# Attention: the denominators of a head in one addition on GpSimd and one inversion on VectorE

## The reference

```python
mask = q_bucket[:, :, :, None] == k_bucket[:, :, None, :]
scores = scale * np.matmul(q, k.transpose(0, 1, 3, 2))
scores = np.where(mask, scores, -1000000000.0)
scores = scores - np.max(scores, axis=-1, keepdims=True)
attn = np.exp(scores)
attn = attn / (np.sum(attn, axis=-1, keepdims=True) + 1e-09)
return np.matmul(attn, v).astype(np.float32)
```

## Time and profile before

| | us |
|---|---|
| median of 3 runs | 746.81 (746.05 to 746.90) |
| the profiled execution | 748.6 |
| its span | 746.8 |
| TensorE, busy in the span | 720.7 (97%) |
| VectorE | 570.9 (76%) |
| ScalarE | 499.9 (67%) |
| GpSimd | 320.1 (43%) |

### The profile page before, as it was taken

How to read it: one execution, slowest core, us unless ns; L and a number is a source line. 1 busy time by engine, 2 the same in 40 slices (tenths; PEclk the granted TensorE clock), 3 DMA queues, 4 the chain that set the end, 5 groups by cost and what they waited for, 6 DMA issues and landing times. The chain is left out here.

```text
span 746.8 us, 13137 instructions
## 1 busy us (share of the span) xinstructions
PE 720.7 (97%) x4017; PEld 608.5 (81%) x4017; DVE 570.9 (76%) x944; ACT 499.9 (67%) x916; POOL 320.1 (43%) x289
## 2 busy tenths in 40 slices
PE   5999999999999989999999999999999999999996
PEld 4889888989998768888888878778887888878884
DVE  6989999999999665629993181498888787887874
ACT  6878788888887653549993272566666656666562
POOL 7767566778741460000000000055454754557543
PEclk9999999999999999999999999999999999999999
DMA  3811111104133368418992000132322423225221
GB/s 128 289 48 39 57 37 47 59 18 160 40 119 128 104 183 285 166 66 313 353 366 84 0 29 0 29 109 88 92 104 85 153 100 100 99 86 169 84 81 60
DMA packets 40532, 85.05 MB, mean 114 GB/s; under 512 B 5585, under 2 KB 9841, under 8 KB 40497
## 3 DMA queue, kind: packets, MB, share of 16 engines
q1 hardware_dynamic: 37776, 77.01, 30.3%
q0 software_dynamic: 2000, 6.98, 2.9%
q10 hardware_dynamic: 720, 0.64, 0.2%
HBM read 76.82 MB, written 6.68 MB: 112 GB/s over the span
## 5 line engine op out<-in xcount | busy, mean ns | idle before, releaser
L601 POOL TENSOR_TENSOR hres<-hexp,hres 128x512 f32<-128x512 f32 x46 | 59.6, 1297 | 305.7 <-DVE hres L1268 305.7
L668 ACT ACTIVATE pTh<-psA 128x384 fp32r<-128x384 f32 x192 | 83.9, 491 | 39.3 <-PE psA L1376 39.0
L949 DVE TENSOR_TENSOR pTl<-psA,pTh 128x384 fp32r<-128x384 f32 x192 | 97.7, 551 | 9.3 <-ACT pTh L668 8.3
L1370 PE MATMUL psA<-K,Q 128*128 128x384 f32 x384 | 92.9, 365 | 3.7 <-ACT K L705 1.7
L942 DVE TENSOR_SCALAR_CACHE_REDUCE psA<-psA 128x768 f32<-128x768 f32 x96 | 91.9, 957 | 3.7 <-PE psA L1370 3.7
L659 ACT ACTIVATE probs<-psA,negmax 128x768 f32<-128x768 f32 x96 | 87.3, 910 | 2.9 <-DVE psA L942 2.5
L1222 DVE TENSOR_TENSOR wil<-rawi,wih 128x512 fp32r<-128x512 f32 x48 | 79.2, 1651 | 6.6 <-ACT wih L787 6.6
L859 ACT ACTIVATE habs<-psA 128x512 f32<-128x512 f32 x48 | 28.7, 598 | 76.8 <-PE psA L1632 74.8
L1206 DVE SCALAR_TENSOR_TENSOR hTl<-psA,hTh 128x512 fp32r<-128x512 f32 x32 | 21.5, 689 | 73.6 <-ACT hTh L767 73.3
L1376 PEld LDWEIGHTS psA<-ident_r,probs_bits 128*128 128x128 f32 x576 | 59.6, 144 | 17.1 <-issue 7.5
L604 POOL TENSOR_TENSOR hsum<-hsum,hres 128x512 f32<-128x512 f32 x46 | 69.7, 1514 | 8.2 <-POOL hres L601 8.2
(11 more groups left out here) (243 smaller groups left out, 1661.1 us busy)
## 6 DMA issues: line engine op xcount, KB each, us to landing
w2s<-in_moe_w SPq DMA_DIRECT2D x9, 2048.0 KB, 10.1
w1s<-in_moe_w SPq DMA_DIRECT2D x9, 2048.0 KB, 10.3
rawi<-in_moe_w_in SPq DMA_DIRECT2D x48, 256.0 KB, 2.6
rawo<-in_moe_w_out SPq DMA_DIRECT2D x48, 256.0 KB, 2.7
raw<-in_qk SPq DMA_DIRECT2D x16, 384.0 KB, 3.2
vs<-in_v SPq DMA_DIRECT2D x16, 192.0 KB, 2.4
x_rows<-X SPq DMA_DIRECT2D x1, 1728.0 KB, 6.8
x_rows<-X SPq DMA_DIRECT2D x1, 1512.0 KB, 5.5
```

Source lines behind the costliest of these rows:

```text
L668: nc.scalar.activation(pTh[u // TPGR % 2][:, g * TPH:(g + 1) * TPH, u % TPGR * P:(u % TPGR + 1) * P], psA[2][:, g, 0:HALF].rearrange("p (t ...
L949: V.tensor_tensor(pTl[u // TPGR % 2][:, g * TPH:(g + 1) * TPH, cols], psA[2][:, g, 0:HALF].rearrange("p (t n) -> p t n", t=TPH), pTh[u // ...
L1370: last = T.matmul(psA[u % 2][:, h, 0:HALF], qs[par][:, cols], ks[par][:, h * HALF:(h + 1) * HALF], start=start, stop=not start)
```

## The change

`den` and `inv` get six columns. GpSimd adds 1e-9 to a head's six sums in one instruction, `denominators`, after `split_qk` of the head two further on (within `prepare`, so between L506 and L474); for heads 13 and 14 it stands at the end of GpSimd's attention work. It waits for the exponentials, for its own split, and for the inversion of the head before. VectorE waits for it and inverts six numbers in the first of a head's two normalisations; the second one only multiplies. For head 15 VectorE does the addition itself. The semaphore `den_step` gives way to `den_ready` and `inv_ready`.

```diff
-        den = sb("den", [P, TPGR])
-        inv = sb("inv", [P, TPGR])
+        den = sb("den", [P, TPB])
+        inv = sb("inv", [P, TPB])
@@ gpsimd
+            def denominators(i, par, before):
+
+                wait_reg(exp_done, i * TPB + TPB)
+                wait_reg(k_split, before)
+                if not (type(i) is int and i == 0):
+                    wait_reg(inv_ready, i)
+                pool.tensor_scalar(den[:, :], sums[:, par * TPB:(par + 1) * TPB], 1e-9, None, ALU.add).then_inc(den_ready, 1)
+                wait_reg(den_ready, i + 1)
+
             def prepare(i, par):
                 split_qk(i, par)
+                if not (type(i) is int and i < 2):
+                    denominators(i - 2, par, i + 1)
                 scale(i + 1, 1 - par)
                 split_v(i, par)
...
             split_qk(HEADS - 1, 1)
+            denominators(HEADS - 3, 1, HEADS)
             split_v(HEADS - 1, 1)
+            wait_reg(v_split, HEADS)
+            denominators(HEADS - 2, 0, HEADS)
@@ vector, normalise
-                dve.wait_ge(exp_done, G * TPGR + TPGR)
-                V.tensor_scalar(den[:, :], sums[:, gm * TPGR:(gm + 1) * TPGR], 1e-9, None, ALU.add).then_inc(den_step, 1)
-                dve.wait_ge(den_step, G * 2 + 1)
-                V.reciprocal(inv[:, :], den[:, :]).then_inc(den_step, 1)
-                dve.wait_ge(den_step, G * 2 + 2)
+                if type(G) is int and G == PAIRS - 2:
+                    dve.wait_ge(exp_done, HEADS * TPB)
+                    V.tensor_scalar(den[:, :], sums[:, TPB:2 * TPB], 1e-9, None, ALU.add).then_inc(den_ready, 1)
+                head = G // 2 if type(G) is int else (G - gm) // 2 + gm // 2
+                if gm % 2 == 0:
+                    dve.wait_ge(den_ready, head + 1)
+                    V.reciprocal(inv[:, :], den[:, :]).then_inc(inv_ready, 1)
+                    dve.wait_ge(inv_ready, head + 1)
                 dve.wait_ge(out_done, G + 1)
                 V.tensor_tensor(X[:, n:n + TPGR, bass.ds(col, XROW)],
                                 ps7[:, 0:TPGR * XROW].rearrange("p (t d) -> p t d", d=XROW),
-                                inv[:, :].unsqueeze(2).broadcast_to([P, TPGR, XROW]), ALU.mult).then_inc(x_ready, 1)
+                                inv[:, gm % 2 * TPGR:(gm % 2 + 1) * TPGR].unsqueeze(2).broadcast_to([P, TPGR, XROW]), ALU.mult
+                                ).then_inc(x_ready, 1)
```

More of the change, by code:

```diff
@@ L249, in build @@
         out_done = sem("out_done")
-        den_step = sem("den_step")
+        den_ready, inv_ready = map(sem, ("den_ready", "inv_ready"))
         x_ready = sem("x_ready")
```

## The result

The changed kernel took 749.1 us (748.1 to 749.5, eleven runs) against 746.8 (745.6 to 747.4, eleven runs) of the kernel before: ratio 1.0026, 95% interval 1.0017 to 1.0034. So it is slower by 0.26%, 1.9 us, a little above what this kernel's measurement can tell from no change, and 0.4 us from the forecast of 748.7. The profiled execution took 749.25 us, with a span of 747.5.

What follows compares the result with a forecast made beforehand. TensorE was taken to set attention's pace, with VectorE close behind. Gain -2.7, head 9's stall +3.6 and the clock's fall 1.2 made +2.1 us on 746.81: 748.9, rounded down to 748.7 us; range 745.8 to 750.5.

Steps and rivals of the forecast that it cites:

- The first halves' gain: Attention, each head's first normalisation: without the add before the inversion, TensorE's hash-to-second-scores distance becomes 3.0 us; gain 2.7 us.
- The second halves' nothing: Attention, each head's second normalisation: VectorE's saved time goes into waiting for ScalarE's cast, distance stays 5.06 us; gain zero.
- Head 9: Its sums stand behind GpSimd's gate block and head 11's split: product 3.8 us late, loss 3.6 us (3.2 to 4.1).
- The clock: After head 9's stall, TensorE's 3.2 us idle makes the granted clock fall to half (6 in 10); cost 1.2 us.
- The end: Head 15, where VectorE adds six sums itself: its last product waits 2.26 us for TensorE anyway, so zero.
- A: Rival: head 9 stalls but the clock stays full, +0.9 us, 747.7 us; chance 0.30.
- B: Rival: shorter second halves pay like the first, 4.1 us more back, 744.8 us; chance 0.07.
- C: Rival: VectorE's inversion waits for GpSimd as the add did, +5 us, near 755 us; chance 0.06.
- D: Rival: the sums are never late, as the block or head 11's split runs sooner, -2.7 us, 744.1; chance 0.05.

Runs made afterwards that it cites:

- the kernel that relieves them alone: The kernel before, with VectorE adding and inverting all six sums in a head's first half and only multiplying in the second: 747.7 us, ratio 1.0005.
- the earlier cast: The changed kernel with sums of heads 0 to 13 ahead of GpSimd's split, and ScalarE's cast of the next K one slot earlier: 741.0 us, ratio 0.9918.
- the cast of one column: The changed kernel with sums of heads 0 to 13 ahead of the split, casting one column of K instead of 768 from head 2 on: 728.2 us.
- my first try: ScalarE's cast of K put behind its slot's two high parts: 747.5 us with head 9's sums added early in the changed kernel, 751.6 in the kernel before.
- the shorter waits: The changed kernel with head 9's sums added inside the split of head 11: behind L500 744.6 us, ratio 0.9973; behind L503 745.7 us, ratio 0.9984.

## Why the prediction came out right, and where it did not

**The first halves' gain** was put at 2.7 us (2.0 to 3.3). The changed trace gives 1.94 + 0.34 + 0.49 + 0.38 = 3.15; the kernel without the addition gives 3.7 by the ratio. Stretch by stretch the terms of the sum were 1.80 for heads 1 to 7, 0.21 for head 8, 0.35 for heads 10 and 11, and 0.36 for the rest. The first three are each short by 0.13 to 0.14 us, mainly since a distance of 3.0 us was taken for every head, and 2.92 to 2.96 came in all but head 1 (3.05). The mechanism was right: the removal of the addition alone gives the gain, and the additions' rows show what held them.

**The second halves' nothing** was right: 5.05 us in the changed kernel, and 5.06 in the kernel that relieves them alone. That ScalarE's cast is what holds them was right too, as the earlier cast and the cast of one column show. Which place would free it was wrong in my first try.

**Head 9.** The sum was to be ready 0.6 us after L506's end; it was 0.84, because the gap before the addition is 0.60 us here, while in steady heads it is 0.29. And VectorE is ready 3.2 us earlier than before, while L506 ends only 3.0 earlier. So the wait is 4.57 instead of 4.07 us. TensorE's hash comes 3.73 us late (against an undisturbed head) where 3.3 was forecast, its idle stretch is 3.67 against 3.2. Behind the hash the sum had another 0.3 us, for VectorE's lateness in the next two slots; the head behind the shorter waits was 0.57 and 0.58 us longer at full clock. If the long wait costs the same there, the stall is worth 4.3 us, against 3.6 forecast (3.2 to 4.1): the mechanism is the one that was told, the term was too small.

**The clock** is the other step that was mis-sized. The fall came in the profiled execution, as put at 6 in 10; in the other ten it can't be placed, only their mean clocks, never above 0.997, are on record. The price was 1.2 us and at most 1.7, from a half-clock stretch of 3.4 us; here the stretch is 6.8 us, and the second head loses 2.33 us. With 0.57 of that for VectorE's lateness, 1.8 us are left for the clock; if the lateness is hidden behind the slower TensorE, all 2.3. The bound was wrong, because it took the one length that the trace showed for the longest possible.

**That the number came out** is partly luck. The gain was 0.45 us larger than the term, stall and clock together 6.06 us instead of 4.8: net 2.9 us lost in attention by the traces, where the sum had 2.1 and the medians say 2.3 (1.9 by the ratio). Errors of opposite sign shrank each other, and between 2.9 and 2.3 lie waits and falls of the clock elsewhere in the launch that differ from one execution to the next, as the two profiles show ahead of and behind attention.

**The end** cost nothing, as said. **The rivals:** A (clock full) fell with the trace of after; B with the kernel that relieves the second halves; C with sixteen inversions of 178 to 191 ns, twelve of which ran wholly beside an L474 (the one at 116.83 from 116.25 to 118.38), as the earlier row had suggested; D with the 4.57 us. The Trainium skill (SBUF — State Buffer, section "SBUF: two separate sides") has the shared ports held for the whole of an instruction, against VectorE where it runs in a two-port mode or reads two SBUF inputs. The 22 held additions agree with it; the one at 31.08, which took 0.16 us beside L474, doesn't. The inversion reads one SBUF input and was never held; whether it runs in such a mode no row shows.

What stays open: why the gap before GpSimd's addition is 0.60 us at head 9 and 0.29 in the steady heads, why the half-clock stretch was 6.8 us in one trace and 3.4 in another, and why the addition at 31.08 was not held. None was tried.

## What to carry to other kernels

A small operation can be moved to a less busy engine only if the place in that engine's queue is right at every iteration: one iteration with a longer queue in front (here a block on the gate) can cost more than fifteen others bring, and its price is read from the row of what will stand ahead of it. Ask first whether the operation is needed, and which of the two in the chain is the slow one: here the addition cost all and changed nothing, while halving the number of inversions brought nothing that can be seen. When an engine that isn't the bottleneck holds a stretch, move its work into an idle stretch of its own timeline, not merely away from the place where it hurts.

## What the runs showed of the hardware

- GpSimd's addition on 128x6 takes 0.23 to 0.27 us. VectorE's inversion takes 155 to 178 ns for three columns and 176 to 193 for six, beside a running GpSimd instruction too.
- VectorE's addition on 128x3 takes 0.15 to 0.17 us alone. Begun beside a GpSimd instruction with more than 0.02 us to go, it ended 0.01 to 0.04 us after that one, in 22 cases of 23, and so took up to 0.80 us; on 128x6 it took 0.45 to 0.72 us so, except where GpSimd's instruction was nearly over.
- Within the launch (its last 10 us left out) the granted clock fell after idle stretches of TensorE of 1.70 us, 2.72 and 3.67 us; in the profiles of the other kernels after 1.93 (the earlier cast), 2.06, 2.10, 2.32 and 2.33 us. In two of these eight it did so only 1.4 and 1.1 us after the work had started again. It stayed at half for 3.4 us in six of the eight and for 6.8 us in two, behind 3.67 and 2.32 us. Behind idle stretches of 1.0 to 1.5 us it didn't fall, nor behind those of up to 2.15 us in the first 10 us of a launch.
- A wait of VectorE up to 0.8 us ahead of head 9's product was free for TensorE's hash; from there it counted one for one.
